# Rows of v added on GpSimd, and the first tile's value products taken by halves, in a fused attention and MLP kernel

## What is computed

```python
# q, k, v: 4 batches, 8 heads, 576 positions, 64 wide; factor = 4
q_d = q.reshape(B, H, 144, 4, D).mean(axis=3)        # k_d, v_d alike
out_d = softmax(q_d @ k_d.T / 8) @ v_d               # pooled attention
out_up = repeat(out_d, 4, axis=2)
scores = where(|i - j| < 4, q @ k.T / 8, -1e9)
out_local = softmax(scores) @ v                      # band attention, 7 keys a query
x = (out_up + out_local) as 2304 rows of 512
x = x / sqrt(mean(x * x) + 1e-6) * rms_g
x = (silu(x @ w_gate) * (x @ w_val)) @ w_out         # 512 -> 1536 -> 512
y = s * relu(x @ w2_in) ** 2 + b;  return y @ w2_out # 512 -> 2048 -> 512
```

## Time and profile before

| | us |
|---|---|
| three runs, median | 982.69 |
| lowest, highest | 978.68, 987.60 |
| the profiled execution | 984.85 |
| its span on the core | 982.9 |

### The profile page before, as it was taken

One profiled execution on the slowest core, in us unless ns is written; L12 is line 12 of the kernel. 1 busy time (PEld: TensorE's weight loads), 2 busy tenths in 40 slices (PEclk: granted clock), 3 DMA queues, 4 the chain that ended last, 5 costly groups with the idle time before them and its releaser, 6 DMA issues.

```text
span 982.9 us, 13208 instructions
## 1 busy us (share of the span) xinstructions
PE 949.1 (97%) x5008; PEld 766.3 (78%) x5031; DVE 537.4 (55%) x813; ACT 354.0 (36%) x816; POOL 368.4 (37%) x192
## 2 busy tenths in 40 slices
PE   7888899989999999999999999999999999999998
PEld 4677699756777777777778998888888888888897
DVE  6888997886775765564542224444433443343343
ACT  2448854752324232422241444222322322222232
POOL 4757866777783876465600454000000000000000
PEclk9898799999999999999999999999999999999999
DMA  9898673433331331012003341102001100100010
GB/s 244 217 259 253 180 216 94 147 87 104 97 111 35 86 106 48 15 38 70 19 9 120 130 129 64 43 1 86 1 1 43 43 0 1 65 1 1 1 43 22
DMA packets 54379, 79.42 MB, mean 81 GB/s; under 512 B 9836, under 2 KB 37068, under 8 KB 52908
## 3 DMA queue, kind: packets, MB, share of 16 engines
q1 hardware_dynamic: 52284, 71.53, 24.8%
q10 hardware_dynamic: 2032, 7.05, 1.9%
HBM read 67.05 MB, written 11.50 MB: 80 GB/s over the span
## 4 chain that ended last, share of the span: by engine, by line
PE 78%; DVE 6%; DMA 4%; POOL 3%; ACT 3%; issue 2%; SPq 2%; ACTq 0%; DVEq 0%; POOLq 0%
PE bank L782 23%; PE bank L922 7%; PE bank L923 7%; PE bank L924 7%; PE bank L905 7%; PE bank L906 7%; PE bank L904 7%; PE bank L818 4%; PE bank L816 4%; PE bank L817 4%; POOL prod L551 3%; DMA rawv<-in_v_dram 2%; ACT prod_a L578 1%; DMA vs<-in_v_dram 1%; PE bank L726 1%
## 5 line engine op out<-in xcount | busy, mean ns | idle before, releaser
L551 POOL TENSOR_TENSOR prod<-qs,ks 128x896 f32<-128x896 f32 x80 | 177.7, 2244 | 89.7 <-DVE sc L596 62.9
L565 POOL TENSOR_TENSOR prod<-sc,vs 128x896 f32<-128x896 f32 x72 | 136.7, 2001 | 64.8 <-DVE x L606 32.7
L945 DVE SCALAR_TENSOR_TENSOR r<-bank,r 128x512 f32<-128x512 f32 (+1 forms) x80 | 51.1, 638 | 181.0 <-ACT r L933 181.0
L906 PE MATMUL bank<-y_h,w2i_l 128*128 128x512 f32 (+1 forms) x320 | 117.7, 368 | 0.0
L933 ACT ACTIVATE r<-bank 128x512 f32<-128x512 f32 (+1 forms) x80 | 44.4, 555 | 181.9 <-PE bank L906 181.2
L838 DVE TENSOR_TENSOR bank<-bank,u 128x512 f32<-128x512 f32 (+1 forms) x66 | 39.6, 599 | 118.0 <-PE bank L782 113.0
L782 PE MATMUL bank<-x_h,wv_h 128*128 128x512 f32 (+1 forms) x264 | 100.0, 390 | 0.0
L596 DVE TENSOR_REDUCE sc<-prod 128x14 f32<-128x896 f32 x80 | 85.7, 1078 | 18.0 <-POOL prod L551 18.0
L816 PE MATMUL bank<-h_h,wo_h 128*128 128x512 f32 (+1 forms) x264 | 93.1, 353 | 0.0
L818 PE MATMUL bank<-h_h,wo_l 128*128 128x512 f32 (+1 forms) x264 | 92.6, 351 | 0.0
L817 PE MATMUL bank<-h_l,wo_h 128*128 128x512 f32 (+1 forms) x264 | 92.5, 351 | 0.0
(11 more groups left out here) (142 smaller groups left out, 1935.7 us busy)
## 6 DMA issues: line engine op xcount, KB each, us to landing
raww<-in_moe_w_out_dram SPq DMA_DIRECT2D x14, 512.0 KB, 4.1
ks<-in_k_dram SPq DMA_DIRECT2D x16, 280.0 KB
vs<-in_v_dram SPq DMA_DIRECT2D x16, 280.0 KB, 5.0
y_scr<-y_st ACTq DMA_DIRECT2D x4, 1024.0 KB, 5.7
raww<-in_moe_w_in_dram SPq DMA_DIRECT2D x8, 512.0 KB, 3.5
y_raw<-y_scr SPq DMA_DIRECT2D x4, 1024.0 KB, 4.8
out_dram<-o_st SPq DMA_DIRECT2D x16, 256.0 KB, 2.8
rawq<-in_q_dram SPq DMA_DIRECT2D x3, 1152.0 KB, 15.2
```

The source lines that it names most:

```text
L551: pool.tensor_tensor(dst, qv, kv, ALU.mult).then_inc(prod_ready, 1)
L565: pool.tensor_tensor(dst, pv, vv, ALU.mult).then_inc(prod_ready, 1)
L906: last = pe.matmul(o, w2i_l[:, m, kk, :], y_h[t % 2][:, kk, 0:w], start=False, stop=kk == DT - 1)
```

## The change

Six things are changed together.

1. `pool_v` runs on POOL, in two halves of eight 72-row blocks (g = 0, 1) for each of batches 1 to 3, and writes into `dv` itself. `vd`, `store_vd`, `load_dv` and the DRAM tensor between them go. `load_rawv(b, g)` loads the halves in the 72-partition layout into two buffers, and for b > 1 waits until `pool_v` has read the one before.
2. The windows of v of tile 0 get eight buffers (`vs3` is new), so their loads wait for no product.
3. `PRODUCTS` takes tile 0's value products by halves: all even n, then all odd n.
4. The root of tile 0 is made twice, for slices 0 and 1 and for 2 and 3 (`inverse_root0(dve, pair)`, 15 instructions each); `normalise` for slices 2 and 3 waits for the second.
5. The lists of all five engines around the first steps are in a new order. On DVE `least(27)` to `least(31)` stand among other calls, three value sums of tile 0 and the second add stand behind the split of the first chunk, and the first sum of tile 1 behind step 0.
6. On SP weight pieces stand further ahead among the windows of tile 1.

```diff
-PRODUCTS = [("qk", 0, n) for n in range(16)] + [("pv", 0, n) for n in range(16) if n not in ACT_PV[0]] + [("qk", 1, n) for n in range(16)]
+HALVES = [n for half in range(2) for n in range(half, 16, 2)]
+PRODUCTS = [("qk", 0, n) for n in range(16)] + [("pv", 0, n) for n in HALVES if n not in ACT_PV[0]] + [("qk", 1, n) for n in range(16)]
...
-        def inverse_root0(dve):
-            dve.wait_ge(sq_ready, FAC)
-            dve.wait_ge(ctr_evac, UNITS * B)
-            a_link(dve, dve.tensor_reduce(CTR[:, 0:FAC], over(sqs[:, 0:], [[1, FAC], [1, 1]]), op=ALU.add, axis=AX.X))
-            inverse_root(dve, CTR)
+        def inverse_root0(dve, pair):
+            dve.wait_ge(sq_ready, 2 * pair + 2)
+            a_link(dve, dve.tensor_scalar(smax[:, 0:2], sqs[:, 2 * pair:2 * pair + 2], 1.0 / E, 1e-6, ALU.mult, ALU.add))
+            inverse_root(dve, smax, 2 * pair, 2)
...
-        def pool_v(eng, b):
-
-            eng.wait_ge(rawv_loaded[b], 16)
-            rv = rawv[b]
-            eng.tensor_tensor(rv[:, :, 0:2 * D], rv[:, :, 0:2 * D], rv[:, :, 2 * D:4 * D], ALU.add).then_inc(v_half[b], 1)
-            eng.wait_ge(v_half[b], 1)
-            wait(eng, vd_stored, 16 * (b - 1))
-            eng.tensor_tensor(vd[:, :, :], rv[:, :, 0:D], rv[:, :, D:2 * D], ALU.add).then_inc(v_pooled[b], 1)
+        def pool_v(pool, b, g):
+
+            rv = rawv[g][0:JH, :, :]
+            n = 2 * (b - 1) + g
+            pool.wait_ge(rawv_loaded[g], 16 * b)
+            pool.tensor_tensor(rv[:, :, 0:2 * D], rv[:, :, 0:2 * D], rv[:, :, 2 * D:4 * D], ALU.add).then_inc(v_half, 1)
+            pool.wait_ge(v_half, n + 1)
+            wait(pool, cpv, H * (b - 1))
+            pool.tensor_tensor(dv[0:JH, b % 2, H * g:H * (g + 1), :], rv[:, :, 0:D], rv[:, :, D:2 * D], ALU.add).then_inc(v_pooled, 1)
...
+                wait(sp, v_pooled, 2 * (b - 2) + g + 1 if b > 1 else 0)
+                sp.dma_start(rawv[g][0:JH, :, :], rows).then_inc(rawv_loaded[g], 16)
...
             qk_mult(pool, 0, 9)
+            pool_v(pool, 1, 0)
+            pool_v(pool, 1, 1)
             qk_mult(pool, 0, 10)
...
-            store_vd(act, 2)
...
-            normalise(act, (2, 3), 1)
+            normalise(act, (2, 3), 2)
...
             load_qk(sp, 1, 7)
+            load_piece(sp, 13)
             load_qk(sp, 2, 0)
-            load_piece(sp, 12)
-            load_piece(sp, 13)
```

More of the change, by code:

```diff
@@ L240, in build @@
         at = [gl_start]
-        rawv = [None] + [place(at, f"rawv{b}", [P, QT, FAC * D], F32) for b in (1, 3)]
+        rawv = [place(at, f"rawv_half{g}", [P, H, FAC * D], F32) for g in range(2)]
+        at = [gl_start + 2 * QT * FAC * D * 4]
         vs2 = place(at, "vs2", [P, 2, WIN * D], F32)
@@ L319, in build @@
         qk_loaded = [sem(f"qk_loaded{i}") for i in range(WSLOTS0)]
-        v_loaded = [sem(f"v_loaded{i}") for i in range(WSLOTS0)]
+        v_loaded = [sem(f"v_loaded{h}") for h in range(H)]
         prod_ready, prod_used = sem("prod_ready"), sem("prod_used")
@@ L1287, in _ @@
             exponents(8)
-            store_vd(act, 1)
             keep_pooled(1, 3)
@@ L1594, in _ @@
             qk_reduce(dve, 0, 6)
-            pool_v(dve, 1)
             qk_reduce(dve, 0, 7)
@@ L1615, in _ @@
             least(15)
-            pool_v(dve, 2)
             least(16)
```

271 lines of the change are left out of this document (138 added, 133 removed).

## The result

| | before | after |
|---|---|---|
| runs side by side, median us | 984.29 | 1005.96 |
| lowest to highest | 978.68 to 987.60 | 1003.73 to 1008.05 |
| the profiled execution, its span | 984.85, 982.9 | 1007.89, 1006.0 |

The changed kernel is slower: ratio 1.0252, 95% interval 1.0219 to 1.0286, some 21.7 us (23.1 between the two spans). The forecast was 988, the range 975 to 996, so the result lies outside it, 10 us beyond its upper end. "Slower by over 1%" had 0.22.

A forecast was written before the change was run, and what follows sets the result against it. The end was taken as P plus 43.5 us to the root's end plus TensorE's remaining work. The first step's -4.5 us was lost in waiting, P's +5.5 us went through: 990.3 profiled, 988 as median, range 975 to 996.

The forecast's parts named there:

- Slower by over 1%: Whole kernel: chance that the change ends over 992.5 us, B and a little of the forecast, 0.22.
- What bounds the kernel: End of the kernel: set by when tile 1's probabilities are ready, plus 43.5 us to the root's end and TensorE's remaining work.
- P: Time when tile 1's probabilities are ready on DVE: 168.5 us before, forecast 174, 5.5 us later.
- The rows of v on POOL: Adds of v moved to POOL: 22 us more POOL, 10.9 us less DVE, 3 us lost on the pooled chain.
- The pooled chain: Stretch up to the first step: ACT sets it, DVE gives up some 9 us, first step near 118 for 122.6.
- Behind the first step: DVE's list after the first step: late tile-0 work puts the first sum of tile 1 at 131 us.
- From 131 to P: Tile 1's sums on DVE: 36.2 us busy, 38 to 40 to the maximum, then exponent and norm; P at 174.
- A: Rival, faster: the front gain carries through, first sum of tile 1 near 124, likeliest 978 us; chance 0.25.
- C: Rival, nothing to measure: the two terms cancel, P within 1.5 us, 983 us; chance 0.14.
- B: Rival, slower beyond 1%: weight pieces on SP delay windows of tile 1, P at 180 or more, 994 us; chance 0.20.

The follow-up runs named there:

- kernels 1 to 12: Twelve follow-up kernels, each the kernel before or the changed kernel with parts of the change added, undone or reordered; 986.0 to 1024.1 us.
- b3: Kernel before with POOL held until DVE has made the low part of weight 16; 977.7 us, ratio 0.9973.
- kernel 2: Kernel before with the rows of v added by DVE straight into dv, no trip through DRAM, old order of all engines; 986.0 us, ratio 1.0032.
- kernel 1: Kernel before with only the rows of v moved to POOL, no trip through DRAM, old order otherwise; 994.4 us, ratio 1.0119.
- kernel 3: Changed kernel with the rows of v added by DVE instead of POOL, all else of the change kept; 1006.8 us, ratio 1.025.
- kernels 9 and 11: 9: kernel before with the new order of tile 1, 998.7 us; 11: the same with tile 1's first two sums back ahead of the first step, 989.3 us.
- kernels 4 and 6: Changed kernel with SP's order of tile 1 altered: 4 puts windows ahead of weight pieces, 1024.1 us; 6 puts pieces ahead of windows, 1007.1 us.

## Why the prediction was wrong, point by point

**What bounds the kernel: right.** The end is P plus a constant. P to step 15 was to stay at 43.5 and measured 42.5, and the table's last column holds over 44 us of P in kernels 1 to 12. b3 shows the other half of it: 4.2 us gained between P and step 15, at an unchanged P, arrive in the span as 4.8 (in the medians as 2.7, for the profiled execution of before is a long one).

**The rows of v on POOL: right in size, wrong in what it decides.** The pieces took 2.36 and 1.26 us (2.35 and 1.27 forecast; one of the short ones 2.26) and all of them 22.7 (22), the minimum of head 11 came at 55.51 (56). The rule of the Trainium skill, GPSIMD Engine Reference, section Engine selection, that such adds belong on VectorE is borne out on the old lists, by 8.4 us (11.0 less 2.6). That 10.9 against 22 us looked like the page's factor of 2 is in part an accident: the new halves have 9216 elements a partition in all, the old adds 5184. The same adds in the same layout took 14.8 us on DVE (kernel 2) and 23.0 on POOL (kernel 1), a factor of 1.6; the 1024-element adds among them 1.24 and 2.37 us each, 1.9. In the changed kernel it is not what loses (kernel 3).

**The pooled chain: the first step that failed.** I had ACT set it, with DVE's 9 us less as pure relief, and put the last exponents of head 31 at 113 and the first step at 118. They came at 121.4 and 125.1. From 72.1 to 117.5 us ACT was busy only 35.24 us and DVE 35.01 (38.85 and 41.99 before), so neither set it by its work. What stands in the trace in its place are waits of the lists for each other: POOL waited 3.42, 3.78, 3.69 and 3.01 us for value sums that stood between heads, DVE waited 2.80 us for ACT's fourth value product ahead of the minimum of head 29, and the first add took 4.20 us beside POOL, where I had only the 1.25 us of before. The gain of 4.5 us became a loss of 2.4. The first add in the kernel before, then the two rows after:

```profile
103.04 1.25 DVE L649 TENSOR_TENSOR x<-x,ct 128x1024 f32<-128x1024 f32 x1
```

```profile
97.93 4.20 DVE L661 TENSOR_TENSOR x<-x,ct 128x1024 f32<-128x1024 f32 x1
...
114.22 1.08 DVE L600 TENSOR_REDUCE x<-prod_a 128x128 f32<-128x896 f32 x1 [2.80 <-ACT prod_a L590]
```

**Behind the first step: right in size.** Forecast 118 to 131, 13 us; measured 125.1 to 138.5, 13.4. "I take the middle" for weights 3 and 2, 4.4 us, met 3.11 and 1.21.

**From 131 to P: the term that was mis-sized.** 43 us forecast, 54.5 measured. Up to the end of the maximum I had DVE busy 36.2 us and took 38 to 40 for the interleaving, so 2 to 4 us of idle DVE. It was 51.7 us (138.5 to 190.2), DVE busy 39.26 of them and idle 12.4 (columns as in the earlier trace rows):

```profile
138.50:190.20 51.70, 41.69 (x322) 38.93 (x320) 39.26 (x61) 16.82 (x32) 34.46 (x16) 0.93 0.50 148
```

So 3.1 us of the difference are DVE work that I priced too low, two-input operations beside POOL among it (weights 9 and 10: 1.80 and 3.12 us, 2.35 for both forecast), and 9 us are idle time. The last piece, exponent and norm, took 2.8 us for the 4 forecast. My allowance leaned on a stretch of the kernel before in which DVE idled 5 us, and was below even that. There six sums were done already, POOL was ahead, and its finished products bridged DVE's waits for TensorE and ACT. Of the 12.4 us here, DVE stood 6.3 behind ACT (2.99 for weight 8, 2.48 for the high part of the turned x) and 5.4 behind POOL; in the earlier trace rows it stood 0.6 and 4.5. That the missing stock of finished sums is why fits this and kernels 9 and 11, but how much each wait would cost with a stock wasn't measured. Kernels 9 and 11 measure tile 1's order apart from the rest of the change: 18.5 us for the whole new order of tile 1, 9.0 with two of its sums back ahead. A better estimate was in the trace of before, from the first sum of tile 1 at 115.2 to P at 168.5: 53.3 us for the whole series, which my sum had shrink to 43. It is 52.4 in kernel 9 (129.0 to 181.45), 54.5 in the changed kernel, 55.6 in kernel 3. Had I moved that stretch as a whole behind my 131, P would have been 184.3, 15.8 later than before, and the forecast 998. Part of that agreement is luck: the series of before holds 47.0 us of DVE work in its 53.3, that of the changed kernel 42.0 in 54.5. And the sum still lacks what came late ahead of 131.

**Sum and rivals.** P was 24.5 us later, not 5.5: 7.1 from the first step, 0.4 behind it, 11.5 from the row of tile 1, and 5.5 were forecast. A (gain carries) needed the first sum of tile 1 near 124 us; it came at 138.5. C fell with it. B had the sign and named 994 or more, and one of its marks, POOL waiting for windows of k, is there with 6.4 us; but nothing shows its mechanism as the cause: kernels 4 and 6 move windows and pieces of the changed kernel both ways, and neither gains. What SP's new order alone costs on DVE's old list was not run.

## What to carry to other kernels

When two in-order engines hand work to and fro through two buffers, price a moved series by its whole measured length in the trace, waits included, and not by the busy time of either engine. Here sixteen products and sums took 50 to 56 us in seventeen kernels, for 33 to 36 us of busy time forecast. Kernels 4 (63.3) and 11 (63.8) show the limits: late weights stretch it, and so does a start with two sums after which the third waits. Causes did not add here (11.0 for POOL's rows, 18.5 for the new order of tile 1, up to 8.5 for the halves, 21.7 together), so undo parts one by one from both kernels before giving any of them a share. And look which engine works beside each two-input operation on the critical list: holding POOL for 4 us, at a place where it is early, was the only kind of edit that beat the kernel before.
